# Attention and two gated layers on one core: keys by a second queue, and five reorderings on GpSimd, VectorE and ScalarE

## The chip, the cores and the metric

One core of a Trainium2 chip runs the whole program. Its engines are TensorE (PE: matrix products and transposes), VectorE (DVE), ScalarE (ACT), GpSimd (POOL) and SyncE (SP, which here only issues transfers). Each engine works through its own instructions in order and waits on semaphores that others raise. The metric is the device time of one execution in microseconds.

## The reference

Three stages. The first is attention over 2 batches, 8 heads, 768 positions, head size 64, with a mask by hash buckets: queries and keys are multiplied by a 64x6 matrix, the six signs are a bucket number, and a query sees only the keys of its own bucket.

```python
mask = q_bucket[:, :, :, None] == k_bucket[:, :, None, :]
scores = scale * np.matmul(q, k.transpose(0, 1, 3, 2))
scores = np.where(mask, scores, -1000000000.0)
attn = softmax(scores)          # minus its maximum, divided by its sum + 1e-9
x = np.matmul(attn, v)          # then (B, S, H*D): 1536 rows of 512
```

The second and the third are two layers on these 1536 rows; the first has 1536 hidden columns, the second 2048.

```python
gate = 1.0 / (1.0 + np.exp(-(x @ w_gate)))
x = (gate * (x @ w_val)) @ w_out
h = x @ w_in
g = np.where(h >= 1, h, np.where(h <= -1, 0.0, (h + 1) ** 2 / 4))
out = g @ w_out2
```

## The kernel before

**Precision.** TensorE multiplies in a rounded fp32. Every operand is therefore split in a rounded high part and the low rest, and each product is high x high, high x low and low x high: three matmuls for one.

**Attention.** The 16 heads go in 8 pairs (index `i`, 0 to 7), each pair in 12 steps (`u`, 0 to 11) of 128 queries; `g` counts all 96 steps. A step makes the scores (TensorE, L702 and L705), evacuates them with their minimum (VectorE, `evacuate`, L1207), takes the exponential (ScalarE, L910), and, three steps at a time, adds epsilon to the sums (GpSimd, `sums`, L486), takes reciprocals (VectorE, L1212) and scales (GpSimd, `normalise`, L491). Then TensorE turns the probabilities (L714), ScalarE takes the high part (L906), VectorE the low one (`low_probs`, L1218), and TensorE weighs the values (L731, L732). On VectorE the reciprocals stand between an evacuation and `low_probs`. Queries and keys of a pair are loaded to `qn` and `kn` (`load_q`, `load_k` on SP), turned by TensorE (`turn`, L665), split in high and low parts (ScalarE L898, VectorE L1185 and L1190), and their signs are found by matmuls (`signs`, L678 to L680). At the start `keep_busy` (L830) puts transposes of the identity between these steps. In the later pairs GpSimd also does work for the first layer ahead of time, one portion at a given step: `first_set` (split of the weights of set 0, at u = 11 of pairs 1 to 6) and `first_sum` (sums of blocks of x into `early`, L567 to L575, in pairs 5 and 6).

**The layers** use Strassen's seven products for four: a *set* `n` is 256 hidden columns for one batch, and `product(n, r)`, r = 0 to 6, are its seven products of six matmuls 128x384 (L748 to L750). There are 40 sets: 0 to 23 are the first layer (even: gate, odd: value), 24 to 39 the second (hinge); groups begin at sets 0, 12, 24 and 32 (`FIRSTS`). Each group has its own seven operands `xop`, made from x by ScalarE (`round_x`), VectorE (`rest_x`) and, for the sums of blocks, `sum_x` (VectorE, L1239 to L1250), which `sum_ahead` spreads over sets of the group before. Products go to two PSUM banks in turn: `product(n, r)` waits until product r - 2 is emptied. ScalarE empties product 0 (`first_product`, copy to u1, L986), VectorE the others (`empty(n, r)`, L1275 and L1282).

**Between the products** TensorE does the down projection of earlier hidden tiles, one piece of it per call of `down()` (L773 to L790), so many after each product as `units(n, r)` says: none in the first set of a group, none for r = 0 to 3 of sets 25 and 33 and then 2, 2 and 4; in a gate set one behind each of products 3 to 6; in set 26 two behind products 0 and 1 and one behind products 2 and 3. In sets 11 and 23 twelve come behind product 6. A tile's first piece waits for its high half `hh` (ScalarE, `round_tile`, L978) and low half `hl` (VectorE, `rest_tile`, L1286). In set 26, the pieces behind products 0 and 1 belong to the last tile of set 24, and the piece behind product 2 is the first of set 25's own tiles.

**Hinge sets.** For each tile VectorE clamps (`clamp`, L1313), ScalarE does relu and square (L996, L999), VectorE adds (`add_hinge`, L1317).

**Weights.** For each set SP loads the raw weights to one of two halves of `stage` (`load_w`), GpSimd makes the Strassen sums (`sums_a`, `sums_b`, L504 to L511), ScalarE rounds (`round_w`), GpSimd takes the low rest (`low_a`, `low_s`, L516 to L522). The narrow weights of the down projection come in pieces through a third, single part of `stage`: `load_wo` (SP), `round_wo` (ScalarE, L960, waits for `wo_in`), `low_wo` (GpSimd, L529, raises `wo_split`). There are 6 pieces in the first layer and 8 in the second, numbers 0 to 13. SP loads a piece only when `low_wo` of the piece before it is through:

```python
if WO2 < n <= WO2 + T2 and n % 2 == 0:
    f = (n - WO2 - 1) // 2
    sp.wait_ge(wo_split, T1 // 2 + f)
    load_wo(wo2_v, f)
```

WO2 is 15, T2 is 16 and T1 is 12, so for n = 26 this is f = 5, piece 11, and it waits for `wo_split` to be 11, that is for `low_wo` of piece 10. ScalarE rounds piece 11 at the end of `round_w` in set 25 (`round_wo2(25)`), ahead of `hinge_part` of tile t of that set.

## Time and profile before

| | |
|---|---|
| median of 3 runs | 792.86 us (792.75 to 793.1) |
| the profiled execution | 792.82 us, its span 790.7 us |
| PE busy | 775.2 us (98%) |
| PEld | 717.3 us (91%) |
| DVE | 551.3 us (70%) |
| ACT | 461.5 us (58%) |
| POOL | 538.5 us (68%) |
| share of the chain that ended last | PE 79%, DVE 6%, ACT 6%, issue 4%, POOL 4% |

The span runs from the first to the last recorded instruction. An engine's idle time counts only where another engine, in the end TensorE, waits for it. In a row of the timeline, what stands in brackets is the engine's idle time just before the instruction, and who ended it. The end of a matmul is modelled, so the distance between two starts tells more than the idle time.

### The profile page before, as it was taken

To read this page: it belongs to the slowest core of one execution; us is meant where nothing else is said; L and a number is where in the kernel's file an instruction comes from. 1 tells how busy PE (TensorE), PEld (TensorE's weight loads), DVE (VectorE), ACT (ScalarE), POOL (GpSimd) and SP (SyncE) were. 2 spreads that over 40 slices of the span, in tenths; PEclk is the share of its full clock that TensorE was granted. 3 is DMA by queue.
4 is the path that set the end of the run, shared out by engine and by line. 5 is a ranking of instruction groups with operands and counts; after the bars stand their busy time and mean duration, and the time that the engine had idled before them with its cause. 6 is when DMAs were issued, how large, how long until landed. Compare 5 with 4: busy or idle time off the path is not lost.

```text
span 790.7 us, 12182 instructions
## 1 busy us (share of the span) xinstructions
PE 775.2 (98%) x4403; PEld 717.3 (91%) x4403; DVE 551.3 (70%) x862; ACT 461.5 (58%) x731; POOL 538.5 (68%) x533
## 2 busy tenths in 40 slices
PE   7999999999999999999999999999999999999998
PEld 6899999998989999999899999988899988899996
DVE  5888888888888666555765655577677776766554
ACT  4888988988997443344453334356455465634443
POOL 4567667778889988877596977747756755465420
PEclk9999999999999999999999999999999999999999
DMA  6895586385100222022021211121121011201002
GB/s 146 181 197 131 136 168 141 79 163 131 55 1 1 80 81 81 29 78 80 27 81 54 80 54 63 44 80 54 32 77 54 29 51 40 95 27 54 1 1 80
DMA packets 61930, 60.08 MB, mean 76 GB/s; under 512 B 28384, under 2 KB 51632, under 8 KB 61872
## 3 DMA queue, kind: packets, MB, share of 16 engines
q1 hardware_dynamic: 61712, 59.32, 28.5%
q8 instruction: 35, 0.57, 0.3%
q14 instruction: 23, 0.19, 0.1%
q10 hardware_dynamic: 160, 0.00, 0.0%
HBM read 37.75 MB, written 3.15 MB: 52 GB/s over the span
## 4 chain that ended last, share of the span: by engine, by line
PE 79%; DVE 6%; ACT 6%; issue 4%; POOL 4%; DMA 0%; SPq 0%; DVEq 0%; POOLq 0%; ACTq 0%
PE ps L748 12%; PE ps L749 11%; PE ps L750 11%; PE ps L777 8%; PE ps L789 5%; PE ps L790 5%; PE ps L788 5%; PE ps L778 4%; PE ps L714 4%; ACT ph L906 2%; PE ps L731 2%; PE ps L732 2%; PE ps L702 2%; DVE probs L1207 2%; PE ps L705 2%
## 5 line engine op out<-in xcount | busy, mean ns | idle before, releaser
L748 PE MATMUL ps<-xop,wset 128*128 128x384 f32 x560 | 191.0, 341 | 4.1 <-DVE u L1282 2.1
L749 PE MATMUL ps<-xop,wset 128*128 128x384 f32 x560 | 189.3, 338 | 0.0
L750 PE MATMUL ps<-xop,wset 128*128 128x384 f32 x560 | 188.8, 337 | 0.0
L1282 DVE TENSOR_TENSOR u<-ps,u 128x384 f32<-128x384 f32 x144 | 79.6, 553 | 109.0 <-PE ps L750 108.3
L516 POOL TENSOR_TENSOR wset<-stage,wset 128x512 fp32r<-128x512 f32 x39 | 56.5, 1448 | 112.7 <-ACT wset L953 112.7
L748 PEld LDWEIGHTS ps<-xop,wset 128*128 128x128 f32 x560 | 105.2, 188 | 18.0 <-issue 3.8
L1218 DVE TENSOR_TENSOR pl<-ps,ph 128x768 fp32r<-128x768 f32 x96 | 91.5, 954 | 26.5 <-ACT ph L906 25.4
L749 PEld LDWEIGHTS ps<-xop,wset 128*128 128x128 f32 x560 | 105.4, 188 | 3.5
L491 POOL TENSOR_SCALAR probs<-probs,small 128x768 f32<-128x768 f32 x96 | 88.4, 927 | 24.9 <-DVE small L1212 22.1
L750 PEld LDWEIGHTS ps<-xop,wset 128*128 128x128 f32 x560 | 105.2, 188 | 0.0
L522 POOL TENSOR_TENSOR wset<-wsum,wset 128x1024 fp32r<-128x1024 f32 x39 | 95.3, 2443 | 0.0
L1207 DVE TENSOR_SCALAR_CACHE_REDUCE probs<-ps 128x768 f32<-128x768 f32 x96 | 90.9, 949 | 5.2 <-PE ps L705 4.6
L910 ACT ACTIVATE probs<-probs,small 128x768 f32<-128x768 f32 x96 | 90.0, 937 | 7.7 <-DVE probs L1207 7.4
L906 ACT CAST ph<-ps 128x768 fp32r<-128x768 f32 x96 | 76.7, 800 | 21.4 <-PE ps L714 19.9
L714 PE MATMUL ps<-ident,probs 128*128 128x128 f32 x576 | 78.9, 273 | 2.1 <-DVE probs L1207 1.2
L1282 DVE TENSOR_TENSOR hid<-ps,u 128x384 f32<-128x384 f32 x84 | 46.6, 555 | 46.8 <-PE ps L750 45.2
L790 PE MATMUL ps<-wo,hl 128*128 128x512 f32 x192 | 75.3, 392 | 0.0
L714 PEld LDWEIGHTS ps<-ident,probs 128*128 128x128 f32 x576 | 67.2, 140 | 9.0 <-issue 3.8
L789 PE MATMUL ps<-wo,hh 128*128 128x512 f32 x192 | 75.3, 392 | 0.0
L777 PE MATMUL ps<-hh,wo 128*128 128x512 f32 x192 | 75.2, 397 | 0.0
L788 PE MATMUL ps<-wo,hh 128*128 128x512 f32 x192 | 74.9, 390 | 0.0
L986 ACT COPY u<-ps 128x384 f32<-128x384 f32 x40 | 19.1, 478 | 93.7 <-PE ps L750 93.7
(134 smaller groups left out, 1710.4 us busy)
## 6 DMA issues: line engine op xcount, KB each, us to landing
stage<-in_moe_w_in_dram SPq DMA_DIRECT2D x16, 512.0 KB, 3.6
stage<-in_moe_w_out_dram SPq DMA_DIRECT2D x14, 512.0 KB, 3.6
stage<-in_moe_w_gate_dram SPq DMA_DIRECT2D x12, 512.0 KB, 4.3
stage<-in_moe_w_val_dram SPq DMA_DIRECT2D x12, 512.0 KB, 3.5
ops<-qh SPq DMA_DIRECT2D x15, 384.0 KB, 5.3
ops<-kh SPq DMA_DIRECT2D x28, 192.0 KB, 5.1
qn<-in_q_dram SPq DMA_DIRECT2D x16, 192.0 KB, 4.5
kn<-in_k_dram SPq DMA_DIRECT2D x16, 192.0 KB, 5.0
```

Of the source, the lines that this page charges most:

```text
L522: pool.tensor_tensor(weights(n, 1)[:, 3:7], wsum[:, :], weights(n, 0)[:, 3:7].bitcast(F32), ALU.subtract).then_inc(w_split, 1)
L714: last = pe.transpose(dst[:, t * P:(t + 1) * P], probs[n % RING][:, t * P:(t + 1) * P], ident[:, :])
L748: pe.matmul(dst, high[:, c, :], high_x(r)[:, c, :], start=(c == 0), stop=False)
L749: pe.matmul(dst, high[:, c, :], low_x(r)[:, c, :], start=False, stop=False)
L750: last = pe.matmul(dst, low[:, c, :], high_x(r)[:, c, :], start=False, stop=(c == 1))
L777: pe.matmul(main, w[:, cols], h[:, t % 3, 0:512], start=(first and n == 0), stop=(last_tile and n == 2))
L788: pe.matmul(ps[:, r, :], hh[:, t % 3, rows], wh, start=first, stop=False)
L789: pe.matmul(ps[:, r, :], hh[:, t % 3, rows], wl, start=False, stop=False)
L790: last = pe.matmul(ps[:, r, :], hl[:, t % 3, rows], wh, start=False, stop=last_tile)
L906: act.copy(dst, turned_slot("T", n).rearrange("p (t n) -> p t n", t=T)).then_inc(pt_high, 1)
L1207: dve.tensor_scalar(probs[g % RING].rearrange("p (s n) -> p s n", s=2), score_slot(g), NO_MATCH, None, ALU.min, ALU.min, accum_out=lowest( ...
L1282: dve.tensor_tensor(dst, bank(n, r), other, ALU.add).then_inc(e_dve, 1)
```

## The change

1. Start: `load_k(0)` on SP issues only the first head's keys; the second head's are issued on ScalarE's queue, after the two transfers of proj. `keep_busy(5)` between the turning of queries and keys becomes `keep_busy(2)`.
2. Pair 5, GpSimd: the three calls of `first_sum` move from steps 4, 7, 10 to 1, 4, 7. What runs at step 4 remains the full sum (k = 0).
3. First layer, VectorE: `sum_ahead` acts at sets 4, 6 and 8 of groups 0 and 1 (it was 3, 4 and 5), and value sets call it no longer; group 2 keeps 3, 4, 5.
4. Sets 1, 11, 13 and 23, VectorE: `gate_second` (768 columns) is two multiplies of 384 columns, one ahead of `empty(n, 5)`.
5. Sets 24 and 32: ScalarE does `first_product(n + 1)` after the square, not between relu and square; VectorE does `add_hinge(t)` ahead of `empty(n + 1, 1)`.
6. GpSimd: `low_wo` of piece 10 runs after set 26's weights; before, after set 25's.

```diff
@@ -351,7 +351,8 @@
             def load_k(i):
                 if i:
                     sp.wait_ge(k_turned, i)
-                for xx in range(2):
+
+                for xx in range(2 if i else 1):
                     sp.dma_start(kn[:, :, xx, :], kv[2 * i + xx]).then_inc(k_in, 16)
 
             def load_v(h):
@@ -626,8 +627,8 @@
                 if 1 <= i < 7 and u == 11:
 
                     first_set(i - 1)
-                if i == NP - 3 and u in (4, 7, 10):
-                    first_sum(0 if u == 4 else 2, (u - 7) // 3)
+                if i == NP - 3 and u in (1, 4, 7):
+                    first_sum(0 if u == 4 else 2, u // 7)
                 if i == NP - 2 and u in (4, 7, 10):
                     first_sum(1 if u == 4 else 3, (u - 7) // 3)
                 if i == NP - 1 and u % 3 == 1:
@@ -649,7 +650,8 @@
                 if n % 2 == 0 and n <= N1 // 2:
                     f = n // 2 - 1
                     low_wo(f, f, (narrow(2 * f + 1), narrow(2 * f)))
-                if WO2 + 1 < n <= WO2 + T2 + 1 and n % 2:
+                if WO2 + 1 < n <= WO2 + T2 + 1 and (n % 2 and n != N1 + 1 or n == N1 + 2):
+
                     f = (n - WO2 - 2) // 2
                     low_wo(T1 // 2 + f, f, (narrow2(2 * f), narrow2(2 * f + 1)))
 
@@ -831,7 +833,7 @@
 
             keep_busy(14)
             turn("Q", 0)
-            keep_busy(5)
+            keep_busy(2)
             turn("K", 0)
             pe.wait_ge(setup, 5)
             signs(0, False)
@@ -991,16 +993,10 @@
                     act.wait_ge(*emptied(n, 6 - second))
                     act.activation(hidden(pp, second), hidden(pp, second), ACT.Sigmoid).then_inc(sig_done, 1)
 
-            def hinge_relu(t):
+            def hinge_part(t):
                 act.wait_ge(clamped, t - TILES1 + 1)
                 act.activation(tile(t), tile(t), ACT.Relu, bias=minus_one).then_inc(hinge_parts, 1)
-
-            def hinge_square(t):
                 act.activation(tmp[:, :], tmp[:, :], ACT.Square, bias=half, scale=0.5).then_inc(hinge_parts, 1)
-
-            def hinge_part(t):
-                hinge_relu(t)
-                hinge_square(t)
 
             def empty_y(g):
 
@@ -1052,15 +1048,11 @@
             def hinge_set(n):
                 t, g = 2 * pair_of(n), group_of(n)
                 ahead = n + 1 in FIRSTS
-                if n - 1 not in FIRSTS:
-                    first_product(n)
+                first_product(n)
                 if n in FIRSTS:
                     round_w(n + 1)
                     empty_y(g - 1)
-
-                    hinge_relu(t)
-                    first_product(n + 1)
-                    hinge_square(t)
+                    hinge_part(t)
                     return
                 round_tile(t - 2)
                 hinge_part(t - 1)
@@ -1085,6 +1077,7 @@
 
             act.dma_start(projn[0:D, :], proj).then_inc(proj_in, 16)
             act.dma_start(projn[D:P, :], proj).then_inc(proj_in, 16)
+            act.dma_start(kn[:, :, 1, :], kv[1]).then_inc(k_in, 16)
             high_turned("Q", 0)
             high_turned("K", 0)
             act.wait_ge(k_high, 1)
@@ -1300,6 +1293,18 @@
                 dve.wait_ge(*emptied(n, 5))
                 dve.tensor_tensor(two, two, tmp[:, :], ALU.mult).then_inc(gated, 1)
 
+            def gate_half(n):
+
+                two = hidden(pair_of(n), 1)
+                dve.wait_ge(sig_done, 2 * pair_of(n) + 1)
+                dve.wait_ge(*emptied(n, 4))
+                dve.tensor_tensor(two[:, G:S], two[:, G:S], tmp[:, G:S], ALU.mult)
+
+            def gate_other(n):
+                two = hidden(pair_of(n), 1)
+                dve.wait_ge(*emptied(n, 5))
+                dve.tensor_tensor(two[:, 0:G], two[:, 0:G], tmp[:, 0:G], ALU.mult).then_inc(gated, 1)
+
             def gate_first(n):
                 one = hidden(pair_of(n), 0)
                 dve.wait_ge(*emptied(n, 6))
@@ -1318,9 +1323,11 @@
 
             def sum_ahead(n):
 
+
                 g = group_of(n)
-                if g < 3 and n - FIRSTS[g] in (3, 4, 5):
-                    sum_x(g + 1, n - FIRSTS[g] - 3)
+                at = (4, 6, 8) if g < 2 else (3, 4, 5) if g == 2 else ()
+                if n - FIRSTS[g] in at:
+                    sum_x(g + 1, at.index(n - FIRSTS[g]))
 
             def gate_set(n):
                 t, g = 2 * pair_of(n), group_of(n)
@@ -1343,13 +1350,14 @@
                 gate_quarter(n)
                 empty(n, 3)
                 empty(n, 4)
-                sum_ahead(n)
-                empty(n, 5)
                 if n - 1 in FIRSTS or n + 1 in FIRSTS:
 
-                    gate_second(n)
+                    gate_half(n)
+                    empty(n, 5)
+                    gate_other(n)
                     empty(n, 6)
                 else:
+                    empty(n, 5)
                     empty(n, 6)
                     gate_second(n)
                 gate_first(n)
@@ -1392,9 +1400,9 @@
                 if ahead:
                     rest_x(g + 1, 1)
                 empty(n, 6)
+                add_hinge(t)
                 if n in FIRSTS:
                     empty(n + 1, 1)
-                add_hinge(t)
                 clamp(t + 1)
                 if ahead:
                     rest_tile(t)
```

**Piece 10 on GpSimd.** GpSimd's rows from the end of set 25's weights; `wset<-wsum` (L522 before, L523 after) is `low_s`, `wo<-stage` is `low_wo`. Before:

```order
L522 TENSOR_TENSOR wset<-wsum,wset 128x1024 [waits w_high]
L529 TENSOR_TENSOR wo<-stage,wo 128x512 [waits wo_high]
L529 TENSOR_TENSOR wo<-stage,wo 128x512
L504 TENSOR_TENSOR wsum<-stage 128x256 [waits w_split,raw_in0]
L505 TENSOR_TENSOR wsum<-stage 128x256
```

Now:

```order
L523 TENSOR_TENSOR wset<-wsum,wset 128x1024 [waits w_high]
L505 TENSOR_TENSOR wsum<-stage 128x256 [waits w_split,raw_in0]
L506 TENSOR_TENSOR wsum<-stage 128x256
L508 TENSOR_TENSOR wsum<-wsum,stage 128x256 [waits sum_parts]
L512 TENSOR_TENSOR wsum<-stage,wsum 128x256 [waits sum_parts]
L517 TENSOR_TENSOR wset<-stage,wset 128x512 [waits w_high]
L519 TENSOR_TENSOR wset<-stage,wset 128x256
L523 TENSOR_TENSOR wset<-wsum,wset 128x1024 [waits w_high]
L530 TENSOR_TENSOR wo<-stage,wo 128x512 [waits wo_high]
L530 TENSOR_TENSOR wo<-stage,wo 128x512
```

The two operations stand seven rows later, behind three that wait for ScalarE's rounding (`w_high`) in set 25.

**The end of pair 5 on GpSimd**, from step 9 to step 0 of pair 6; `early<-x` is `first_sum`, L540 and L541 (L541 and L542) are `first_set`. Before:

```order
L491 TENSOR_SCALAR probs<-probs,small 128x768 [waits rcp_done,o_done]
L572 TENSOR_TENSOR early<-x 128x384
L491 TENSOR_SCALAR probs<-probs,small 128x768 [waits rcp_done]
L540 TENSOR_TENSOR wset<-wsum,wset 128x512 [waits first_parts]
L541 CAST wset<-wsum 128x512
L486 TENSOR_SCALAR small<-small 128x3 [waits exp_done]
```

Now:

```order
L492 TENSOR_SCALAR probs<-probs,small 128x768 [waits rcp_done,o_done]
L492 TENSOR_SCALAR probs<-probs,small 128x768 [waits rcp_done]
L541 TENSOR_TENSOR wset<-wsum,wset 128x512 [waits first_parts]
L542 CAST wset<-wsum 128x512
L487 TENSOR_SCALAR small<-small 128x3 [waits exp_done]
```

The half sum is gone from here; one stands at step 1 instead.

**ScalarE in sets 24 and 25.** `hid<-hid,small` is relu, `tmp<-tmp,small` the square, `u<-ps` the copy of product 0, `hh<-hid` is `round_tile`. Before:

```order
L996 ACTIVATE hid<-hid,small 128x768 [waits clamped]
L986 COPY u<-ps 128x384 [waits e_dve,p_done]
L999 ACTIVATE tmp<-tmp,small 128x768
L978 CAST hh<-hid 128x768 [waits tile_used,hinge_done]
L996 ACTIVATE hid<-hid,small 128x768 [waits clamped]
```

Now:

```order
L998 ACTIVATE hid<-hid,small 128x768 [waits clamped]
L999 ACTIVATE tmp<-tmp,small 128x768
L988 COPY u<-ps 128x384 [waits e_dve,p_done]
L980 CAST hh<-hid 128x768 [waits tile_used,hinge_done]
L998 ACTIVATE hid<-hid,small 128x768 [waits clamped]
```

The copy of set 25's product 0 and the square have changed places.

## Rows read from the trace of the kernel before

**Rows 1.** page, busy time of each engine over the whole span: us (share) xinstructions
```profile
PE 775.2 (98%) x4403; PEld 717.3 (91%) x4403; DVE 551.3 (70%) x862; ACT 461.5 (58%) x731; POOL 538.5 (68%) x533
```

**Rows 2.** timeline, start: start us, us, engine, line, operation, [idle before <-releaser]
```profile
1.52 3.25 PE L830 MATMUL ps<-ident 128*128 128x128 f32 x14 [1.52 <-POOL ident L463]
6.44 1.23 PE L830 MATMUL ps<-ident 128*128 128x128 f32 x5
7.51 0.82 PE L665 MATMUL ps<-ident,kn 128*128 128x128 f32 x6
10.22 0.44 PE L678 MATMUL ps<-kh,wk_h 128*128 128x384 f32 x1 [0.30 <-DVE kl L1190]
```

**Rows 3.** windows view, 1.5 to 5.0 us: engines busy, granted clock, DMA share, GB/s
```profile
1.50:5.00 3.50, 3.25 (x14) 2.85 (x14) 1.96 (x20) 1.28 (x1) 0.00 (x0) 1.00 0.76 168
```

**Rows 4.** timeline, ends of head pairs 4 and 5: GpSimd and VectorE
```profile
153.38 0.95 DVE L1207 TENSOR_SCALAR_CACHE_REDUCE probs<-ps 128x768 f32<-128x768 f32 x1
156.22 0.95 DVE L1207 TENSOR_SCALAR_CACHE_REDUCE probs<-ps 128x768 f32<-128x768 f32 x1
180.54 1.02 POOL L572 TENSOR_TENSOR early<-x 128x384 f32<-128x384 f32 x1
182.49 0.95 DVE L1207 TENSOR_SCALAR_CACHE_REDUCE probs<-ps 128x768 f32<-128x768 f32 x1
184.56 0.18 DVE L1212 RECIPROCAL small<-small 128x3 f32<-128x3 f32 x1 [1.12 <-POOL small L486]
186.37 0.95 DVE L1207 TENSOR_SCALAR_CACHE_REDUCE probs<-ps 128x768 f32<-128x768 f32 x1
```

**Rows 5.** timeline, TensorE at the ends of value sets 3 and 5
```profile
291.50 0.34 PE L748 MATMUL ps<-xop,wset 128*128 128x384 f32 x1
292.56 0.44 PE L748 MATMUL ps<-xop,wset 128*128 128x384 f32 x1 [0.37 <-DVE u L1282]
316.31 0.44 PE L748 MATMUL ps<-xop,wset 128*128 128x384 f32 x1 [0.24 <-DVE u L1282]
```

**Rows 6.** VectorE by form, 250 to 790 us: xcount | busy us, mean ns | idle
```profile
L1286 DVE TENSOR_TENSOR hl<-hid,hh 128x768 fp32r<-128x768 f32 x56 | 61.6, 1100 | 1.4 <-ACT hh L978 1.4
L1282 DVE TENSOR_TENSOR hid<-ps,u 128x384 f32<-128x384 f32 x84 | 46.6, 555 | 46.8 <-PE ps L750 45.2
L1317 DVE TENSOR_TENSOR hid<-hid,tmp 128x768 f32<-128x768 f32 x32 | 34.2, 1068 | 8.2 <-ACT tmp L999 7.5
L1313 DVE TENSOR_SCALAR tmp<-hid 128x768 f32<-128x768 f32 x32 | 27.1, 846 | 2.3
L1301 DVE TENSOR_TENSOR hid<-hid,tmp 128x768 f32<-128x768 f32 x12 | 14.3, 1194 | 0.1
```

**Rows 7.** timeline, TensorE in hinge sets 25 and 33
```profile
547.22 0.44 PE L748 MATMUL ps<-xop,wset 128*128 128x384 f32 x1 [0.91 <-DVE hid L1282]
673.85 0.44 PE L748 MATMUL ps<-xop,wset 128*128 128x384 f32 x1 [0.56 <-DVE hid L1282]
```

**Rows 8.** GpSimd and SP around set 25, and the landing of SP's load
```profile
540.61 2.84 POOL L529 TENSOR_TENSOR wo<-stage,wo 128x512 fp32r<-128x512 f32 x2
553.54 2.40 POOL L522 TENSOR_TENSOR wset<-wsum,wset 128x1024 fp32r<-128x1024 f32 x1
543.48 0.37 SPq L403 DMA_DIRECT2D stage<-in_moe_w_out_dram  x1
stage<-in_moe_w_out_dram SPq DMA_DIRECT2D x1, 512.0 KB, 3.6
```

**Rows 9.** timeline, sets 25 and 26: ScalarE, VectorE, TensorE
```profile
552.05 1.13 ACT L960 CAST wo<-stage 128x512 fp32r<-128x512 f32 x2
554.88 1.89 DVE L1317 TENSOR_TENSOR hid<-hid,tmp 128x768 f32<-128x768 f32 x1 [0.88 <-ACT tmp L999]
560.82 0.34 PE L748 MATMUL ps<-xop,wset 128*128 128x384 f32 x1
561.88 0.39 PE L788 MATMUL ps<-wo,hh 128*128 128x512 f32 x1
```

## The prediction, made before the changed kernel was timed

> **What bounds the kernel now.** I read first the busy table of the page, then TensorE's idle time in the timeline, and then, around each place that the diff touches, the timelines of the engines there. TensorE is busy for 98% of the span [rows 1], so a microsecond of idle TensorE, wherever it lies, is a microsecond of the kernel, and work on another engine costs something only where TensorE ends up waiting for it. The sum below is therefore a list of TensorE's holes: those that the change closes, and one that it opens. The profiled execution took 792.82 us (its span is 790.7, about 2.1 us lie around it); the median of the three runs is 792.86, so the sum against the one holds for the other. 0.2% (1.6 us) is about what a measurement of this kernel can tell from no change.
>
> **Start: the first keys.** The critical thing here is the sign matmuls of the keys, which wait 0.30 us for the low keys (at 10.22). Today both key transfers are issued behind both query transfers on SP, five filling transposes run from 6.44, and the keys are turned from 7.51 [rows 2]. With two fillers instead of five, at (7.51 - 6.44) / 5 = 0.21 us each, the turn can begin 0.64 us earlier, if the keys have landed. That moves the chain keys turned, ScalarE high part, VectorE low part; but the query's sign matmuls run right up to that 0.30 us hole, so no more than 0.30 us comes back. Against it: the second keys are then in flight beside the second queries, and TensorE turns the queries the moment they are there. The DMA engines moved 168 GB/s from 1.5 to 5.0 us [rows 3]; 196.6 KB at that rate are 1.17 us, the most that the queries can be pushed back. So the start is worth between -0.30 and -0.30 + 1.17 = +0.87 us. I take -0.1, near the end that has a measured hole, because part of the queries is already through when the keys join them. The Trainium skill (DMA: Bandwidth & Descriptors, Issuing engines are not separate DMA queues) says that transfers issued from different engines run on the same DMA engines and interleave, so a second queue saves only issue time. By that rule alone the queries land late and this term would stand at its upper end; no row here shows two queues with large transfers at once.
>
> **Attention, head pair 5 (`first_sum`).** GpSimd is late at the end of this pair: a half sum of 1.02 us at 180.54, then the split of set 0, then the sums of the softmax; VectorE stands 1.12 us waiting for these before its reciprocals, at 184.56 [rows 4], and TensorE behind VectorE. The price is seen between the evacuations: from the one at 182.49 to the next are 3.88 us, where the pair before has 156.22 - 153.38 = 2.84 [rows 4], that is 1.04 us. The change takes the half sum at step 10 out and puts one at step 1, where GpSimd waits for others; steps 4 and 7 keep a sum of the same size each. GpSimd then reaches the softmax sums 1.0 us earlier, nearly in time. Bounds: 0 (something else late) and -1.04. I take **-1.0**.
>
> **First layer, the sums of x (`sum_ahead`).** They leave value sets 3, 5, 15 and 17 for gate sets, where TensorE has a piece of the down projection after each of the later products and VectorE has room. In set 3 GpSimd's sums of weights and VectorE's sums of x get in each other's way, and VectorE comes late to the next set: two matmuls follow in 292.56 - 291.50 = 1.06 us instead of 0.53, a hole of 0.53; in set 5 the idle is 0.24 where the first shows 0.37, so by the same 0.16 between idle and loss some 0.40 [rows 5]. Together **-0.9**; bounds 0 (another contention takes their place) and -1.3 (smaller holes in group 1 go too).
>
> **First layer, the gate product in two halves.** In sets 1, 11, 13 and 23, one multiply of 1.19 us mean (L1301) [rows 6] becomes two of 384 columns, the first ahead of `empty(n, 5)`. In 11 and 23 TensorE has twelve down pieces behind the set: nothing. In 1 and 13 product 6 is emptied right behind. The total is bounded by -0.2 per set (half of it fits into the wait for product 5) and, if a half beside GpSimd's work costs as much as the whole, +1.2 per set. I take +0.1 for both: two halves cost one start more and hide one wait.
>
> **Second layer, the first hinge set of each group.** ScalarE does the square ahead of the copy of the next set's product 0, and VectorE's `add_hinge` comes ahead of `empty(n + 1, 1)`. In set 33 TensorE now waits 0.56 us for `empty(33, 2)` [rows 7], which stands behind `add_hinge` and `clamp`; with the square one copy earlier, that chain ends about 0.5 us sooner. The copy becomes later by the square, and product 2 waits for it, but it ends as that product's turn comes. **-0.5**, bounds -0.6 and +0.4. In set 25, where the same wait is 0.91 us (at 547.22) [rows 7], the like brings about 0.9; it is lost again in the next step and counted there.
>
> **Second layer, piece 10 of the narrow weights (`low_wo`), the term that decides.** GpSimd's low half of piece 10 moves from behind set 25's weights to behind set 26's. That looks free for GpSimd, which waits much. But three in-order queues hang on it. The stage buffer for piece 11 is the same one, so SP's load of piece 11 waits for `wo_split` 11, that is for this very operation; now it is issued at 543.48, the moment GpSimd ends the pair that begins at 540.61 [rows 8]. ScalarE rounds piece 11 in set 25 (`round_wo2(25)`), at 552.05 [rows 9], ahead of `hinge_part` of its own tile and of the copy of set 26's product 0. With the change:
>
> - GpSimd's `low_s(26)` begins at 553.54 and takes 2.40 [rows 8], so it ends at 555.9. It hangs on ScalarE's rounding in set 25, which comes about those 0.9 earlier: 555.0. Piece 10 then takes the 2.84 of its two operations: 557.85.
> - SP issues piece 11, 3.6 us to landing [rows 8]: 561.5. ScalarE, which got there at about 551.1, has stood for some 10 us.
> - From ScalarE's start on piece 11 to VectorE's `add_hinge` are 554.88 - 552.05 = 2.83 [rows 9]: 564.3. At about the same time ScalarE copies product 0 of set 26 (0.5), and TensorE's product 2 of set 26, which needs that bank, starts at 564.8. It starts at 560.82 now [rows 9].
> - The down piece behind it needs the low half of the tile: VectorE does `add_hinge` 1.07, `clamp` 0.85, `empty` 0.55 and `rest_tile` 1.10 by the means [rows 6]; those with GpSimd idle are less, and I take 3.0 in all: 567.3. TensorE takes the piece at 567.4 against 561.88 now [rows 9].
>
> TensorE can do only product 0 and 1 of set 26 and four down pieces meanwhile, and it does them in the order written; so its stream after this is **+5.5** us late, the 0.9 won in set 25 included. Bounds: 564.8 - 560.82 = +4.0 (the low half adds nothing) and +7.0 (the two loads behind each other, means of VectorE as they stand, the next tile late too). Set 27's own piece is rounded a whole set later and has its buffer in time, so the cost comes once.
>
> **The sum:** -0.1 - 1.0 - 0.9 + 0.1 - 0.5 + 5.5 = +3.1; 792.82 + 3.1 = **795.9 us**, slower by 0.4%.
>
> **Rivals.**
> 1. *The clock falls in the hole.* The granted clock is full, 2.4 GHz, in the stretches that I read; of the first 14 transposes, which took 3.25 us or 0.23 each where 6 later ones took 0.82 or 0.137 [rows 2], the view gives it as 1.00 as well [rows 3], but they are as long as the lower level, 1.2 GHz, would make them: about 1.7 times. The new hole of nearly 5 us is longer than any in this trace. If the clock is down for as long as the hole lasted, 5 us do the work of 3: +2, that is 797.9. Nothing here shows a fall; nothing excludes it. The Trainium skill (TensorE: Matmul & The Clock Gate, HAM oscillation) says that a gap without matmuls can bring the slower clock, and that the first work behind it then runs at half rate. No run so far shows it. Chance 0.20.
> 2. *Faster: piece 11 is not waited for.* If its load lands before ScalarE reaches it, the +5.5 is gone and the 0.9 of set 25 stays: 792.82 - 2.4 - 0.9 = 789.5. It decides at 551 us: the piece has to be there then. For it: the same load has 4.9 us in hand today (543.48 + 3.6 = 547.1 against 552.05 [rows 8, 9]). Against it: the operation that frees its buffer comes 14 us later. Chance 0.09.
> 3. *No change:* the hole costs about what the rest brings, 2.4, because ScalarE's stand begins later or more of the down pieces cover it: 792.82 - 2.4 + 2.4 = 792.8. Chance 0.13.
> 4. *The start turns against it:* queries late by the full 1.17, and the split gate products dearer by 1: 798. Chance 0.06.
> 5. *The gains in attention and first layer don't come,* the hole does: 797.8. Chance 0.07.
>
> My forecast has 0.45. **Range** 793.0 to 799.2: from the edge of the no-change case to the clock case with the hole at its upper bound; it leaves out the faster case and part of rival 3. Slower by over 0.2%: 0.45 + 0.20 + 0.06 + 0.07 = 0.78; within: 0.13; faster: 0.09.
>
> **What would show it.** In the profile after: ScalarE's longest wait is for the DMA of piece 11, about 10 us, in set 25; TensorE has holes of some 4.8 and 1.5 us at products 2 of set 26 and the piece behind it; SP issues that load near 554 (all else is about 3 to 4 us earlier by then). The step from evacuation 72 to 73 is 2.9 us instead of 3.88; the holes in sets 3 and 5 are gone. If ScalarE shows no such wait, the reading of the queues is wrong and the kernel is faster; if there is a granted clock under 1 behind the hole, rival 1 holds.

## Result and profile after

The changed kernel takes **801.72 us** (median of 6 runs, 799.08 to 802.05), the kernel before beside it 792.59 (6 runs, 792.25 to 793.1): ratio 1.0107, 95% interval 1.0092 to 1.0121 (the ratios of this document are taken over all the runs, not from the two medians, which here would give 1.0115). By the medians it is slower by 9.1 us; forecast were 3.1, and a range that ended at 799.2. The direction and the place were right, the size was not. The profiled execution took 800.01 us, its span is 798.2: 7.2 us more time and 7.5 us more span than the one of before.

Busy time of the page, changed kernel; it answers to [rows 1]:

```profile
PE 776.4 (97%) x4400; PEld 718.5 (90%) x4400; DVE 557.2 (70%) x866; ACT 460.9 (58%) x731; POOL 537.6 (67%) x533
```

TensorE is busy for about a microsecond more and has 6 us more of idle time. The place, in the timelines of ScalarE, GpSimd, SP, VectorE and TensorE, changed kernel (each engine is its own answer; they answer to [rows 8, 9]):

```profile
560.20 1.14 ACT L962 CAST wo<-stage 128x512 fp32r<-128x512 f32 x2 [9.83 <-DMA stage<-in_moe_w_out_dram]
...
551.76 2.40 POOL L523 TENSOR_TENSOR wset<-wsum,wset 128x1024 fp32r<-128x1024 f32 x1
554.11 2.54 POOL L530 TENSOR_TENSOR wo<-stage,wo 128x512 fp32r<-128x512 f32 x2
...
556.68 0.37 SPq L404 DMA_DIRECT2D stage<-in_moe_w_out_dram  x1
...
563.03 0.96 DVE L1322 TENSOR_TENSOR hid<-hid,tmp 128x768 f32<-128x768 f32 x1 [10.80 <-ACT tmp L999]
...
563.41 0.69 PE L750 MATMUL ps<-xop,wset 128*128 128x384 f32 x1 [4.21 <-ACT u L988]
566.46 0.79 PE L790 MATMUL ps<-wo,hh 128*128 128x512 f32 x1 [0.77 <-DVE hl L1279]
568.23 0.52 PE L751 MATMUL ps<-xop,wset 128*128 128x384 f32 x1
568.55 0.52 PE L752 MATMUL ps<-xop,wset 128*128 128x384 f32 x1
```

Read it in the order in which one releases the next: GpSimd ends piece 10 at 556.65, SP issues piece 11 at 556.68 (it was 543.48 [rows 8]), ScalarE has stood for 9.83 us when it can round it, VectorE 10.80, TensorE 4.21. What is new is in the durations: a 128x384 matmul takes 0.52 instead of the 0.34 of [rows 9]. (The 0.69 and 0.79 are of the first matmul behind a wait, which is longer at full clock too: 0.44 in [rows 7].) The distance between starts tells it best: 568.55 - 568.23 = 0.32 for a 128x384 matmul, where the same pair of matmuls goes at 0.18 once the stretch is over (572.10 and 572.28 in the same timeline). The windows view gives the reason (us, busy of PE, PEld, DVE, ACT, POOL, granted clock, DMA share, GB/s):

```profile
558.00:560.00 2.00, 1.20 (x6) 0.66 (x4) 0.00 (x0) 0.00 (x0) 0.00 (x0) 1.00 0.88 317
560.00:562.00 2.00, 0.00 (x0) 0.00 (x0) 0.00 (x0) 1.80 (x3) 0.29 (x1) 0.88 1.06 374
562.00:564.00 2.00, 0.59 (x2) 0.59 (x3) 0.96 (x1) 1.36 (x3) 2.00 (x3) 0.50 0.25 80
...
568.00:570.00 2.00, 2.00 (x8) 2.00 (x7) 0.25 (x1) 2.00 (x4) 0.45 (x1) 0.50 0.00 0
570.00:572.00 2.00, 2.00 (x8) 1.71 (x7) 1.58 (x2) 0.43 (x1) 2.00 (x2) 0.56 0.00 0
572.00:574.00 2.00, 2.00 (x11) 1.76 (x10) 1.02 (x2) 0.00 (x0) 2.00 (x2) 1.00 0.00 0
```

The clock fell to its lower level, 1.2 GHz, inside the hole, and stayed there until about 571.8, through some 8 us of work.

The other places. Start and attention, changed kernel (they answer to [rows 2, 4]):

```profile
6.57 0.88 PE L667 MATMUL ps<-ident,qn 128*128 128x128 f32 x6 [1.80 <-DMA qn<-in_q_dram]
7.50 0.82 PE L667 MATMUL ps<-ident,kn 128*128 128x128 f32 x6
9.43 0.41 PE L680 MATMUL ps<-qh,wq_h 128*128 128x384 f32 x1 [1.11 <-DVE ql L1178]
...
182.79 0.95 DVE L1200 TENSOR_SCALAR_CACHE_REDUCE probs<-ps 128x768 f32<-128x768 f32 x1
183.90 0.18 DVE L1205 RECIPROCAL small<-small 128x3 f32<-128x3 f32 x1 [0.16 <-POOL small L487]
185.71 0.95 DVE L1200 TENSOR_SCALAR_CACHE_REDUCE probs<-ps 128x768 f32<-128x768 f32 x1
```

The queries came 1.80 us late (0.34 before). The step between the two evacuations is 185.71 - 182.79 = 2.92, as forecast (2.9), where [rows 4] has 3.88. And the gate product of set 1, VectorE, GpSimd and TensorE, with TensorE in set 13 as the last row:

```profile
262.86 1.67 DVE L1301 TENSOR_TENSOR hid<-hid,tmp 128x384 f32<-128x384 f32 x1
265.03 1.04 DVE L1306 TENSOR_TENSOR hid<-hid,tmp 128x384 f32<-128x384 f32 x1
...
261.72 2.39 POOL L523 TENSOR_TENSOR wset<-wsum,wset 128x1024 fp32r<-128x1024 f32 x1
...
265.14 0.41 PE L750 MATMUL ps<-xop,wset 128*128 128x384 f32 x1 [1.01 <-DVE tmp L1275]
266.69 0.41 PE L750 MATMUL ps<-xop,wset 128*128 128x384 f32 x1 [0.26 <-DVE u L1275]
...
407.99 0.41 PE L750 MATMUL ps<-xop,wset 128*128 128x384 f32 x1 [0.66 <-DVE tmp L1275]
```

One half of the product took 1.67 us, more than the whole had by [rows 6] (1.19), and TensorE waited for the emptying of product 5 behind it. That wait is new in both sets.

**Where the time went**, in all profiled executions. I took the start of one recurring instruction, VectorE's emptying of product 2 of each set (and the first evacuation for the start), and its distance to the same one in the kernel before. The table gives how much this distance grew over each place, in us, and in the last column how much the span grew behind set 39; all runs named are explained below.

| | start | attention | set 1 | sets 3, 5, 17 | set 13 | set 24 to 25 | 25 to 32 | 32 to 33 | at set 39 | behind it |
|---|---|---|---|---|---|---|---|---|---|---|
| changed kernel | +0.23 | -0.84 | +1.28 | -1.37 | +0.64 | -1.54 | **+8.88** | -0.65 | +6.48 | +1.04 |
| e1, piece 10 back | +1.01 | -0.96 | +1.21 | -1.36 | +0.62 | -0.05 | 0.00 | -0.66 | -0.53 | +1.15 |
| e2, piece 10 alone | -0.04 | -0.03 | -0.08 | +0.02 | -0.04 | -0.91 | **+8.52** | -0.01 | +7.29 | 0.00 |
| e3, hole filled | -0.55 | -0.97 | +1.28 | -1.34 | +0.63 | -1.56 | **+6.67** | -0.66 | +3.13 | +1.06 |
| e4, rounding later | -0.49 | -0.84 | +1.25 | -1.35 | +0.64 | -1.55 | **+0.79** | -0.63 | -2.33 | +1.06 |
| f2, start alone | +0.72 | +0.15 | -0.02 | +0.05 | 0.00 | -0.02 | +0.05 | -0.02 | +0.99 | 0.00 |
| f4, halves alone | -0.62 | +0.08 | +1.26 | -0.09 | +0.65 | -0.02 | +0.01 | -0.01 | +1.17 | +1.16 |
| g1, sums alone | -0.48 | -0.87 | -0.03 | -1.24 | -0.04 | -0.02 | 0.00 | -0.02 | -2.82 | 0.00 |
| f5, hinge order alone | -0.72 | +0.10 | 0.00 | +0.03 | -0.04 | -0.04 | +0.02 | -0.67 | -1.56 | 0.00 |
| g3, best kernel | -0.58 | -1.10 | -0.07 | -1.30 | -0.03 | -1.57 | +0.02 | -0.64 | -5.43 | +0.01 |

What is missing to the column of set 39 lies between the places and is under 0.4. The start column changes between runs of one kernel (below); those of the sets repeat to about 0.1 wherever the same code runs, and attention to 0.3. In 25 to 32 the runs that leave piece 10 in its place stay within 0.05; the three that round piece 11 later have +0.79 (e4), +0.46 (f1) and +0.02 (g3). So each is a price that can be read off, there to some 0.8.

**The last column** has its 1.0 to 1.2 us only in the five kernels with the halved gate product (changed kernel, e1, e3, e4, f4) and at most 0.01 in all others, f1, f3 and g2 included. It lies in the last store. DMA view of the last microseconds, f4 and then the kernel before:

```profile
q14 instruction: 1, 0.01, 0.5%
...
out_dram<-x SPq DMA_DIRECT2D x1, 256.0 KB, 3.2
...
out_dram<-x SPq DMA_DIRECT2D x1, 256.0 KB, 2.1
```

The last 256 KB land 3.2 us after their issue instead of 2.1, and beside them a packet of instructions is loaded (8 KB, 1.8 to 1.9 us behind the last copy). Both are in the five kernels and neither is in the other nine. So the edit that adds four VectorE operations in the first layer costs another microsecond at the end of the kernel (f4 has it alone). That the packet is what holds the store up is argued from this coincidence; no run moves it alone.

### The profile page after: what moved, and what is told of

Same layout as the page of the kernel before. It is cut to its first block, busy times and chain, and to the rows that moved or that the text cites. A ratio compares the mean times of both kernels' runs of the same rounds, so it can differ in the third digit from the quotient of the medians.

```text
span 798.2 us, 12184 instructions
## 1 busy us (share of the span) xinstructions
PE 776.4 (97%) x4400; PEld 718.5 (90%) x4400; DVE 557.2 (70%) x866; ACT 460.9 (58%) x731; POOL 537.6 (67%) x533
## 4 chain that ended last, share of the span: by engine, by line
PE 78%; DVE 7%; ACT 6%; issue 4%; POOL 3%; DMA 1%; SPq 0%; DVEq 0%; POOLq 0%; ACTq 0%
PE ps L750 12%; PE ps L751 11%; PE ps L752 11%; PE ps L779 8%; PE ps L790 5%; PE ps L792 5%; PE ps L791 5%; PE ps L780 4%; PE ps L716 4%; ACT ph L908 3%; PE ps L733 2%; PE ps L734 2%; DVE probs L1200 2%; PE ps L704 2%; PE ps L707 2%
## 5 line engine op out<-in xcount | busy, mean ns | idle before, releaser
L523 POOL TENSOR_TENSOR wset<-wsum,wset 128x1024 fp32r<-128x1024 f32 x39 | 95.3, 2444 | 0.0
```

What stands on the lines that cost most here:

```text
L523: pool.tensor_tensor(weights(n, 1)[:, 3:7], wsum[:, :], weights(n, 0)[:, 3:7].bitcast(F32), ALU.subtract).then_inc(w_split, 1)
```

## Experiments

Each experiment ran beside the kernel before on the same chip, and its ratio is to those runs.

**e1: the changed kernel with piece 10 back in its place.**

```
-  if WO2 + 1 < n <= WO2 + T2 + 1 and (n % 2 and n != N1 + 1 or n == N1 + 2):
+  if WO2 + 1 < n <= WO2 + T2 + 1 and n % 2:
```

> The changed kernel with low_wo of piece 10 back behind set 25's weights; all else of the change stays. Theory (the late piece 10 is the whole loss, everything else together gains): shifts against the kernel before, read at VectorE's empties of the changed trace, are -0.24 us by set 24 and -1.78 by set 25, and set 32 gives another -0.65, so 792.6 - 2.4 = 790.2 us, with no wait of ScalarE for a DMA in set 25, no TensorE hole over 1.1 us behind the start's 1.8 us, and granted clock 1.0. Rival (the other edits lose as well, the start and the halved gate products above all): 793 us or more.

793.25 us (11 runs, 791.39 to 793.99), ratio 1.0002 [0.9993, 1.0011]. The loss of 9 us is gone, but nothing is won, as the rival had it: set 24 to 25 brings -0.05 instead of -1.54, the halves take 1.8 and another 1.15 in the last store, and this run's start 1.0.

**e2: the kernel before with piece 10 late, and nothing else** (the same line, the other way round).

> The kernel before with this one edit alone: low_wo of piece 10 behind set 26's weights. Theory: the whole loss is here, +8 to +10 us: 800.5 to 802.5 us, ScalarE waiting about 9 us for the DMA of piece 11, a TensorE hole of over 3.5 us at product 2 of set 26, and the granted clock at half behind it. Rival (the hinge order makes the hole, since ScalarE's copy of product 0 stands behind the square): not over 796 us.

800.56 us (4 runs, 800.12 to 800.8), ratio 1.0097 [1.0082, 1.0112]. The loss comes with this one line: 8.3 us, with the hinge order of before, so the rival falls. TensorE, e2:

```profile
564.17 0.69 PE L748 MATMUL ps<-xop,wset 128*128 128x384 f32 x1 [4.45 <-ACT u L986]
567.73 0.79 PE L788 MATMUL ps<-wo,hh 128*128 128x512 f32 x1 [1.28 <-DVE hl L1286]
```

**e3: the changed kernel, the hole filled.** Twenty matmuls of a zero tile ahead of product 2 of set 26 add nothing to the result and keep TensorE at work.

```
+  if n == N1 + 2 and r == 2:
+      for _ in range(20):
+          pe.matmul(ps[:, 0, :], zero[:, :], wo[:, 0, 0], start=False, stop=False)
   product(n, r)
```

> The changed kernel with 20 matmuls of a zero matrix (128x512, added to a running sum, which stays as it is) ahead of product 2 of set 26: 20 x 0.23 = 4.6 us of TensorE work in the hole of 4.2 us. Theory (the hole costs twice: once as lateness, once by the clock that falls to half behind it for 10.2 us): the clock stays at 1.0, product 2 and the piece behind it come at most 0.5 us later than in the changed kernel, and the time falls by 2 to 4.5 us, to 797 to 799.5, with runs within 0.5 us of each other. Rival (the loss behind the hole is the lateness of ScalarE and VectorE themselves, not the clock): 801.5 us or more, as before or longer by the filler.

799.5 us (6 runs, 796.66 to 800.27), ratio 1.0076 [1.006, 1.0092]. Windows view of e3, and TensorE's timeline there:

```profile
560.00:562.00 2.00, 2.00 (x10) 1.65 (x9) 0.00 (x0) 2.00 (x3) 0.00 (x0) 1.00 0.80 276
562.00:564.00 2.00, 1.86 (x10) 1.23 (x8) 1.75 (x3) 1.34 (x4) 0.06 (x1) 1.00 0.12 40
564.00:566.00 2.00, 0.46 (x2) 0.42 (x3) 1.81 (x3) 1.64 (x2) 2.00 (x2) 1.00 0.06 22
```

```profile
557.99 4.70 PE L880 MATMUL ps<-wo,zero 128*128 128x512 f32 x20
565.54 0.49 PE L790 MATMUL ps<-wo,hh 128*128 128x512 f32 x1 [1.68 <-DVE hl L1282]
```

The clock stays at 2.4 GHz, and the place costs 6.67 instead of 8.88: **the fall of the clock is worth 2.2 us, the wait itself 6.7.** The medians say the same, 799.5 for 801.72, though the runs lie 3.6 us apart where 0.5 was expected. The fillers run a little over: counted from set 25, where e3 is at -2.91 and the changed kernel at -1.78, product 2 begins 0.25 us later in e3 (at 562.53, for 563.41). So the wait itself may be up to 0.25 less and the clock's part as much more. The 1.68 us of idle TensorE at 565.54 did not bring it down here.

**e4: the changed kernel, ScalarE rounds piece 11 one set later,** behind its rounding of set 27's weights, so that `hinge_part` and the copy of set 26 no longer queue behind the load.

```
-  if n < WO2 + T2 and n % 2 and not ahead:
+  if n < WO2 + T2 and n % 2 and not ahead and n != N1 + 1:
       round_wo2(n)
+  if n == N1 + 2:
+      round_wo2(n - 1)
```

> The changed kernel, piece 10 still late on GpSimd, but ScalarE rounds piece 11 one set later (in set 26, behind the rounding of set 27's weights). Theory (the loss is only that ScalarE stands in its queue before a load that cannot be there): within 0.5 us of the kernel with piece 10 back, about 790.2 us, no hole in set 26, clock 1.0. Rival (GpSimd's and SP's lateness, the raw weights of set 27 being loaded 13 us later than before, costs by itself): 793 us or more, TensorE waiting for weights of set 27.

791.43 us (12 runs, 790.01 to 792.98), ratio 0.9982 [0.9973, 0.9991]. That is 1.8 us below e1, mostly the gain at set 25 that e1 lacks, and 1.2 above the expected 790.2, which knew nothing of the microsecond in the last store. GpSimd is as late as in the changed kernel, the load too, and the hole is gone; ScalarE rounds piece 11 at 567.48 with no wait. So the in-order queue of ScalarE in front of the load was the cost. What is left for GpSimd's lateness is the +0.79 of the table at most: SP issues the raw weights of set 27 behind piece 11, and ScalarE waits 3.18 us for them here and 1.88 in g3, where the place costs 0.02.

**f2 and f3: the start alone,** on the kernel before: the second keys on ScalarE's queue, f2 with two fillers (the last two lines), f3 with the five of before.

```
-  for xx in range(2):
+  for xx in range(2 if i else 1):
...
+  act.dma_start(kn[:, :, 1, :], kv[1]).then_inc(k_in, 16)
...
-  keep_busy(5)
+  keep_busy(2)
```

> The kernel before with the change's start alone (the second keys on ScalarE's queue, two fillers). Theory: the second keys share the DMA engines with the second queries and these come late, by an amount that differs from run to run (waits of 0.4 to 1.8 us in the runs so far); the whole start is worth between -0.5 and +1.0, the median +0.2: 792.5, runs spread over more than 1.5 us. Rival: the start is a gain of 0.3 at a median run, since the keys' signs no longer wait, and the late queries of the other runs came from elsewhere: 792.0, spread as before's.

> The kernel before with the second keys on ScalarE's queue, and the five fillers kept. Theory (the queue, not the fillers, makes the start vary): the queries wait 0.4 to 1.8 us as in the kernel with two fillers, and five fillers come on top at 0.21 each, so it is 0.3 to 0.6 us slower than that kernel: 792.9. Rival (the fillers count: with two of them TensorE's clock rises later, as it did by 4 us in one run): with five the rise comes where it comes before, and the kernel is as fast as before or faster than the one with two.

f2: 794.19 us (12 runs), ratio 1.0004 [0.9992, 1.0017]. f3: 793.88 (12 runs), ratio 1.0007 [0.9997, 1.0018]. The intervals show no difference from before or from each other, so the fillers' 0.3 to 0.6 us does not appear. Queries wait 1.02 and 1.45 us. The start of f2, and then of the best kernel without the longer filling (f1), whose start is that of the kernel before:

```profile
5.80 1.54 PE L665 MATMUL ps<-ident,qn 128*128 128x128 f32 x6 [1.02 <-DMA qn<-in_q_dram]
7.14 0.63 PE L830 MATMUL ps<-ident 128*128 128x128 f32 x2
7.56 1.49 PE L665 MATMUL ps<-ident,kn 128*128 128x128 f32 x6
```

```profile
5.38 1.54 PE L667 MATMUL ps<-ident,qn 128*128 128x128 f32 x6 [0.60 <-DMA qn<-in_q_dram]
6.72 1.27 PE L832 MATMUL ps<-ident 128*128 128x128 f32 x5
7.78 1.49 PE L667 MATMUL ps<-ident,kn 128*128 128x128 f32 x6
```

Six transposes of keys take 1.49 us in both, and 0.82 in [rows 2] and in the changed kernel: TensorE works at half speed at 7.6 us in two runs and at full speed in two others, whatever the start looks like. The runs show it as two groups. f2 has 4 at 792.4 to 792.8 and 8 at 793.8 to 795.8; the kernel before, in the same chip's 29 runs, 19 at 792.2 to 793.2 and 10 at 794.0 to 796.3. The profiled runs bear it out: six key transposes take 1.43 to 1.49 in e1, f1, f2 and f3, of which e1, f2 and f3 lie in their upper groups (793.12, 793.83, 794.78), and 0.82 to 0.91 in all others, which lie low but for g2.

**f4: the halves of the gate product alone,** on the kernel before.

```
-  empty(n, 5)
...
-  gate_second(n)
+  gate_half(n)
+  empty(n, 5)
+  gate_other(n)
```

> The kernel before with the gate product in two halves and nothing else. Theory: product 5 is emptied a half product later than product 0 of the next set wants its bank, so TensorE waits about 1.1 us longer in set 1 and 0.6 in set 13, nothing in 11 and 23: 792.3 + 1.7 = 794.0 us. Rival: the shift in sets 1 and 13 came from the sums of x that moved to sets 4, 6 and 8 or from elsewhere: then the sets show under 0.3 and the time is that of before.

795.07 us (12 runs, 794.82 to 797.46), ratio 1.0026 [1.0016, 1.0037], and the two prices of the changed kernel again: +1.26 and +0.65. The median is 1.1 above the expected 794.0; the +1.16 behind set 39 had not been seen then. VectorE, GpSimd and TensorE in set 1, f4:

```profile
262.92 1.66 DVE L1308 TENSOR_TENSOR hid<-hid,tmp 128x384 f32<-128x384 f32 x1
...
261.77 2.39 POOL L522 TENSOR_TENSOR wset<-wsum,wset 128x1024 fp32r<-128x1024 f32 x1
...
265.19 0.41 PE L748 MATMUL ps<-xop,wset 128*128 128x384 f32 x1 [0.98 <-DVE tmp L1282]
```

The half starts inside GpSimd's split of weights, which ends at 261.77 + 2.39 = 264.16, and ends itself 0.42 us behind that, at 264.58. The same in the kernel before, where product 5 is emptied ahead of the product:

```profile
264.27 1.29 DVE L1301 TENSOR_TENSOR hid<-hid,tmp 128x768 f32<-128x768 f32 x1
...
262.36 2.39 POOL L522 TENSOR_TENSOR wset<-wsum,wset 128x1024 fp32r<-128x1024 f32 x1
```

GpSimd ends at 264.75, the whole product at 265.56, 0.81 behind: about twice 0.42 for twice the columns. So nearly all of the stall is in the moment of the start: 1.24 us of it for the early half, 0.48 for the whole. The Trainium skill (SBUF — State Buffer, SBUF: two separate sides) says that GpSimd's operations and VectorE's with two inputs in SBUF take a shared pair of ports for the whole instruction, and that the loser is blocked. By that rule the half would begin at 264.16 and take its own time. The shortest half in f4 took 0.56 and the shortest whole product before 0.95, so both rows agree with it to 0.14 us.

**f5: the hinge order alone,** on the kernel before.

```
-  first_product(n + 1)
   hinge_square(t)
+  first_product(n + 1)
...
+  add_hinge(t)
   if n in FIRSTS:
       empty(n + 1, 1)
-  add_hinge(t)
```

> The kernel before with the hinge order alone; piece 10 stays in its old place. Theory: in set 33 TensorE's wait goes (-0.65); in set 25 GpSimd's two operations of piece 10 lie beside VectorE's clamp and take the gain back (0 to +0.2): -0.5 in all. Rival (the order itself gains in set 25, as the shift of -1.5 in the changed kernel suggests, whatever GpSimd does): -0.9 at set 25 and -0.65 at 33, 1.5 in all.

791.3 us (11 runs, 791.07 to 793.18), ratio 0.9989 [0.9981, 0.9998]. -0.67 in set 33, -0.04 in set 25, as the first theory has it. VectorE, GpSimd and TensorE in f5, then VectorE and GpSimd in e4, where piece 10 is away:

```profile
539.88 1.56 DVE L1313 TENSOR_SCALAR tmp<-hid 128x768 f32<-128x768 f32 x1
...
539.72 2.86 POOL L529 TENSOR_TENSOR wo<-stage,wo 128x512 fp32r<-128x512 f32 x2
...
545.30 0.45 PE L748 MATMUL ps<-xop,wset 128*128 128x384 f32 x1 [0.33 <-DVE u L1282]
```

```profile
539.76 0.56 DVE L1320 TENSOR_SCALAR tmp<-hid 128x768 f32<-128x768 f32 x1
...
539.79 1.12 POOL L505 TENSOR_TENSOR wsum<-stage 128x256 f32<-128x256 f32 x1
```

The same `clamp` takes 1.56 us when GpSimd's first half of piece 10 is under way 0.16 us earlier, and 0.56 when it gets in first. This microsecond is what moving piece 10 alone gains at set 25 (e2: -0.91); with the hinge order on top it is -1.54, and the hinge order without it -0.04: the two belong together.

**g1: the sums alone,** on the kernel before: the half sum of attention earlier, the sums of x in gate sets.

```
-  if i == NP - 3 and u in (4, 7, 10):
-      first_sum(0 if u == 4 else 2, (u - 7) // 3)
+  if i == NP - 3 and u in (1, 4, 7):
+      first_sum(0 if u == 4 else 2, u // 7)
...
-  if g < 3 and n - FIRSTS[g] in (3, 4, 5):
-      sum_x(g + 1, n - FIRSTS[g] - 3)
+  at = (4, 6, 8) if g < 2 else (3, 4, 5) if g == 2 else ()
+  if n - FIRSTS[g] in at:
+      sum_x(g + 1, at.index(n - FIRSTS[g]))
```

> The kernel before with the half sum of attention a few steps earlier and the sums of x in the gate sets, and nothing else. Theory: both gains stand by themselves, as the shifts in the changed kernel gave them: -0.96 us in head pair 5 and -0.57 - 0.44 - 0.36 = -1.37 in the sets 3, 5 and 17, in all -2.3, so 790.3 us where before has 792.6. Rival: part of these holes only moved, and is paid at the end of a set that the changed kernel's other edits had made late anyway: then -1.2 or less.

790.4 us (11 runs, 789.7 to 791.8), ratio 0.9976 [0.9967, 0.9984]. -0.87 and -1.24 in the table: these parts stand by themselves.

**f1 and g3: the best of the change.** f1 is e4 with the start of before and the gate product whole; g3 has three more filling transposes ahead of the first queries. g2 is the kernel before with these three. f1 against e4, then the edit of g2 and g3:

```
-  for xx in range(2 if i else 1):
+  for xx in range(2):
...
-  keep_busy(2)
+  keep_busy(5)
...
-  act.dma_start(kn[:, :, 1, :], kv[1]).then_inc(k_in, 16)
...
-  gate_half(n)
   empty(n, 5)
-  gate_other(n)
+  gate_second(n)
```

```
-  keep_busy(14)
+  keep_busy(17)
```

> Theory: what is worth keeping of the change are the early half sum of attention (-0.96 us), the sums of x in gate sets (-1.37) and the hinge order together with piece 10 moved (-1.5 at set 25, -0.65 at set 33); what costs are the start, the halved gate product (+1.1 in set 1, +0.64 in set 13) and ScalarE standing at piece 11 in set 25. This kernel keeps the first three, has the start and the whole gate product of before, and rounds piece 11 a set later. Expected by the theory: 788.5 us, with evacuation 72 to 73 at 2.9, no gap behind the gate of set 1, and no hole at set 26. Rival: the halved product also brought something (the wait for product 5), so that with it gone the sets 1 to 13 show no gain over the run with the change's halves: then 790.5 or more.

> The kernel before with 17 transposes instead of 14 ahead of the first queries, so that TensorE has next to no idle time before these. So far the granted clock reached its upper level at moments between 5 and 10 us into the span, and the runs of each kernel fall in two groups, 1.7 us apart: 17 of 52 runs of the kernel before in the upper one, 22 of 35 of those with the change's start. Theory A: TensorE's idle time ahead of the queries decides which, so with 17 fillers hardly a run is in the upper group (1 or 2 of 12). Theory B: it is a matter of chance: 4 of 12, as before. The lower group stays at 792.3, or 0.2 above where the queries are early.

> The best kernel so far (the changed one with the start and the whole gate product of before, and piece 11 rounded a set later) with 17 fillers. Theory A: 788.4 us median, hardly a run above 789.2. Theory B: as without them, 788.2 to 791.1, median 789.0 to 789.6.

f1: 789.62 us (6 runs, 788.21 to 791.11), ratio 0.995 [0.9935, 0.9965]. g2: 792.04 (12 runs, 2 of them at 794.5 and 794.7), ratio 0.9997 [0.9989, 1.0006]. **g3: 787.67 (5 runs, 787.41 to 787.95), ratio 0.9941 [0.9929, 0.9953], 4.7 us faster than the kernel before** beside it. In f1 the gate product costs nothing in set 1 or behind set 39, so its rival (the halves also brought something) falls; its time is 1.1 above the expected 788.5, with a late start of 0.95. Theory A (idle TensorE ahead of the queries makes the slow starts) is not shown: with 17 fillers 2 of 17 runs were in the upper group (2 of 12 in g2, none of 5 in g3), where the kernel before had 24 of 81 beside the experiments, a difference that chance still gives about once in ten. And g2's own profiled run is one of the two, for another reason. TensorE and ScalarE, g2, two windows of g2, and TensorE in the kernel before:

```profile
19.84 0.84 PE L702 MATMUL ps<-ops 128*128 128x384 f32 x2 [1.88 <-DVE ql L1185]
...
17.99 0.81 ACT L898 ACTIVATE qh<-ps 128x768 fp32r<-128x768 f32 x1 [0.79 <-DMA ops<-ql]
```

```profile
20.00:22.00 2.00, 2.00 (x7) 2.00 (x8) 2.00 (x5) 1.44 (x3) 1.29 (x3) 0.52 0.94 177
22.00:24.00 2.00, 2.00 (x11) 1.91 (x11) 1.43 (x4) 1.24 (x3) 1.51 (x2) 0.63 0.98 241
```

```profile
19.25 0.62 PE L702 MATMUL ps<-ops 128*128 128x384 f32 x2 [0.97 <-DVE ql L1185]
```

ScalarE waited 0.79 for a DMA, TensorE 1.88 instead of 0.97, and the clock was down for about 3.4 us. That is the +1.95 between the start and the first layer in this run; before, at the same wait of 0.97, the clock stayed up.

## Why the prediction was wrong where it was

- **Piece 10: the mechanism was right, the term was not: +7.3 (8.88 - 1.54) for a forecast +5.5.** Each link came: SP's issue (forecast near 554, measured 556.68), ScalarE's stand (some 10 us, 9.83), TensorE's two holes (4.8 and 1.5 us, 4.21 and 0.77). The wait alone is 6.67 in e3 (its second hole is 1.68 there), the forecast 5.5 + 0.9 = 6.4. What failed is the step "the granted clock is full", which kept the clock out of the sum; it stood as rival 1, at +2, with a chance of 0.20, and e3 measures 2.2. That rival's aside on the start was sound: the windows view prints 1.00 from 0 us on in all these runs, also where the transposes go at half speed (the keys' in f2 from 7.56), so ahead of the first rise only the durations tell. The gain in set 25 was 0.6 larger than forecast (1.54 for 0.9), since GpSimd's piece 10 had held up the clamp as well.
- **Gate product in halves: forecast +0.1, measured +1.92 in the sets and about +1.1 more in the last store, 3.0 in all.** This is the second step that failed, and the dearer one. The bound was about right for set 1 (+1.2 per set, "if a half beside GpSimd's work costs as much as the whole"; the half took 1.67 and the set lost 1.28) and I took the other end. The step "two halves cost one start more and hide one wait" did not look at what GpSimd did at the moment to which the half was moved, nor that product 0 of the next set waits for the emptying of product 5, now behind it. The end of the kernel had no term at all.
- **Start: forecast -0.1, bounds -0.30 to +0.87.** The late queries are there, 1.02 to 1.80 us in four of six profiled runs with the new queue (0.49 and 0.38 in the others), beside 0.34 to 0.76 without it and with the same 14 fillers. The four agree with the Trainium skill (DMA: Bandwidth & Descriptors, Issuing engines are not separate DMA queues), by which the transfers of two queues interleave; the other two do not show it. The effect on the time is within what f2 and f3 can tell, -0.1% to +0.2%. What I had not counted is the spread: 17 of the first 52 runs of the kernel before lay in the upper group, and 22 of 35 with the new start (e1, f2 and f3), which chance gives in under one of a hundred (f2 and f3 alone, 15 of 24 for 10 of 29 beside them, in about one of twenty). So the new start probably makes late rises of the clock more frequent, but no run shows how. The difference of medians here holds some of that: 4 of the changed kernel's 6 runs are at 801.69 to 802.05, 2 at 799.08 and 800.01, and the profiled one is among the lower.
- **Attention: right.** -1.0 forecast, -0.96 between the evacuations, -0.87 alone in g1.
- **Sums of x: right, a bit small.** -0.9 forecast, -1.37; set 17 in the other group brings 0.36 that I had left to the bound.
- **Hinge order, set 33: right.** -0.5 forecast, -0.65 (f5: -0.67).

The sum of the measured terms is +0.23 - 0.84 + 1.28 - 1.37 + 0.64 - 1.54 + 8.88 - 0.65 = +6.6; 6.5 of it are there at set 39, and 1.04 come behind it, in the last store: 7.5 of span. The median is slower by 9.1; the rest is that four of the six runs lie 1.7 to 2.0 above the profiled one, which looks like a late rise of the clock, but none of them was profiled. Rival 1 held; with the gate product 3.0 dearer as well it comes to 797.9 + 2.9 = 800.8, near the measured 801.7. The range's upper end is 799.4 by its own sum (797.9 + 1.5) and not 799.2; the measured time lies above both.

## What to carry to other kernels

When an operation of an idle engine is moved, follow what it frees, not what it costs: here 2.5 us of GpSimd's work, moved over GpSimd's idle time, held back a load, and an in-order engine stood in front of that load with everybody's work behind it. If such a load must come late, move its consumer too (e4: from +9.1 to -0.8 us against the kernel before). Price an expected TensorE hole of some 4 us with the time at half clock behind it as well. Before an operation of VectorE on SBUF is moved or split, look at what GpSimd runs at the new moment. And compare the end of the span too: here four operations more came with 1.1 us behind the last set.

## What was not expected of the hardware

- A hole of 4.2 us in a busy TensorE brought the granted clock to 0.5 for 10.2 us in the changed kernel and for 6.8 us in e2 (4.45 us of hole); one of 1.88 us was followed by 3.4 us at 0.5 in g2, and one of 1.68 us in e3 was not, nor one of 0.97 at the place of g2's in the kernel before. What decides beside the length of the hole was not tried.
- The first rise of the clock comes at different moments in runs of the same start: transposes at full speed from 5.26 us in f4, at half speed until behind 7.8 in f1. It comes with up to 1.7 us at the first evacuation (-0.72 in f5 to +0.95 in f1, both with the start of before), as much as the whole of a small change.
- A 128x768 clamp on VectorE took 1.56 us where GpSimd's operation had begun 0.16 us before it (f5), and 0.56 where that began 0.03 us after it (e4).
- The last store landed about 3.2 us after its issue instead of 2.1 in the five kernels in whose last microseconds an 8 KB packet of instructions was loaded.
